# The softmaxed taps of a convolution built on every partition by VectorE instead of by a product, and two convolution steps of the second block placed ahead of the first gated product

## The reference, cut to what matters

```python
w = softmax(weight, axis=-1)               # weight: 8 heads x 7 taps, 1e-9 added to the sum
x = einsum('hk,bskhg->bshg', w, windows)   # out[s] = sum_k w[head, k] * x_pad[s + k]
h = sigmoid(x @ w_gate) * (x @ w_val)      # 192 -> 1536
x = h @ w_out                              # 1536 -> 192
r = maximum(x @ w_in2, 0)                  # 192 -> 2048
out = (r * r) @ w_out2                     # 2048 -> 192
```

## Time and profile before

| | |
|---|---|
| median of 3 runs | 2343.72 us (2342.58 to 2344.52) |
| the profiled execution, its own time | 2343.65 us |
| its span in the trace | 2341.9 us |
| TensorE (PE) busy | 2335.8 us, 100% of the span |
| VectorE (DVE) busy | 1884.9 us, 80% |
| ScalarE (ACT) busy | 1277.3 us, 55% |
| GpSimd (POOL) busy | 156.6 us, 7% |

### The profile page before, as it was taken

One profiled execution on the slowest core, in us unless ns is written; L12 is line 12 of the kernel. 1 busy time (PEld: TensorE's weight loads), 2 busy tenths in 40 slices (PEclk: granted clock), 3 DMA queues, 4 the chain that ended last, 5 costly groups with the idle time before them and its releaser, 6 DMA issues.

```text
span 2341.9 us, 54356 instructions
## 1 busy us (share of the span) xinstructions
PE 2335.8 (100%) x20539; PEld 1929.7 (82%) x20539; DVE 1884.9 (80%) x3968; ACT 1277.3 (55%) x2350; POOL 156.6 (7%) x125
## 2 busy tenths in 40 slices
PE   9999999999999999999999999999999999999999
PEld 7888888888888888888888888888888888888887
DVE  7778878788788787887878878788788787887856
ACT  5645555545554555544555545555555554455556
POOL 3100000000000000000000000000000000000000
PEclk9999999999999999999999999999999999999999
DMA  6111111011110111101111111111111111111101
GB/s 171 44 26 47 29 47 49 25 47 29 49 47 25 47 29 49 47 25 47 39 39 47 35 39 40 36 47 43 31 47 29 47 47 27 47 29 49 41 19 37
DMA packets 93343, 99.28 MB, mean 42 GB/s; under 512 B 8256, under 2 KB 77376, under 8 KB 93312
## 3 DMA queue, kind: packets, MB, share of 16 engines
q1 hardware_dynamic: 92240, 97.81, 16.7%
q10 hardware_dynamic: 1072, 1.05, 0.2%
HBM read 19.27 MB, written 12.58 MB: 14 GB/s over the span
## 4 chain that ended last, share of the span: by engine, by line
PE 99%; DVE 0%; issue 0%; ACT 0%; DVEq 0%; ACTq 0%
PE hp L506 55%; PE acc L571 25%; PE acc L579 17%; PE hp L507 1%; PE acc L572 0%; PE acc L580 0%; PE hp L681 0%; DVE y L1051 0%; PE hp L655 0%; DVE lo L1011 0%; DVE hid_t L997 0%; PE hp L516 0%; PE hp L628 0%; PE acc L671 0%; PE acc L506 0%
## 5 line engine op out<-in xcount | busy, mean ns | idle before, releaser
L506 PE MATMUL hp<-xs,w 64*128 64x512 f32 x5745 | 1394.5, 386 | 0.7 <-DVE hid_t L997 0.5
L507 PE MATMUL hp<-xs,w 64*128 64x512 f32 x5745 | 1394.5, 386 | 0.0
L506 PEld LDWEIGHTS hp<-xs,w 64*128 64x128 f32 x5745 | 1056.8, 184 | 227.3 <-DVE hid_t L997 1.8
L507 PEld LDWEIGHTS hp<-xs,w 64*128 64x128 f32 x5745 | 1056.8, 184 | 0.0
L1011 DVE TENSOR_TENSOR lo<-hid_t,hi 128x512 fp32r<-128x512 f32 x896 | 613.4, 688 | 63.9 <-ACT hi L777 59.8
L807 ACT ACTIVATE act_t<-hp 128x512 f32<-128x512 f32 x383 | 229.5, 599 | 690.4 <-PE hp L506 690.3
L572 PE MATMUL acc<-hi,wo 64*128 64x512 f32 x1788 | 547.7, 386 | 0.0
L571 PE MATMUL acc<-hi,wo 64*128 64x512 f32 x1788 | 547.7, 386 | 0.0
L810 ACT ACTIVATE act_t<-hp 128x512 f32<-128x512 f32 x512 | 302.8, 598 | 186.9 <-PE hp L507 186.8
L997 DVE TENSOR_TENSOR hid_t<-hp,act_t 128x512 f32<-128x512 f32 x383 | 264.4, 690 | 154.9 <-ACT act_t L807 146.6
L571 PEld LDWEIGHTS acc<-hi,wo 64*128 64x128 f32 x1788 | 329.0, 184 | 70.2
(11 more groups left out here) (116 smaller groups left out, 2175.4 us busy)
## 6 DMA issues: line engine op xcount, KB each, us to landing
xs<-xs SPq DMA_DIRECT2D x158, 256.0 KB, 3.8
xs<-y_rest SPq DMA_DIRECT2D x126, 128.0 KB, 3.4
out_dram<-stage SPq DMA_DIRECT2D x31, 384.0 KB, 2.6
xin<-in_x_dram SPq DMA_DIRECT2D x30, 384.0 KB, 3.3
moved<-y_parts SPq DMA_DIRECT2D x32, 128.0 KB, 2.2
moved<-z_parts SPq DMA_DIRECT2D x31, 128.0 KB, 2.2
stage<-in_moe_w_out_dram SPq DMA_DIRECT2D x7, 384.0 KB, 4.7
stage<-in_moe_w_in_dram SPq DMA_DIRECT2D x12, 128.0 KB, 2.8
```

The costliest lines, as they stand in the source:

```text
L506: low = pe.matmul(banks[:, 0, :], w[lower, wk, c], xs[lower, xk, :], start=s, stop=e)
L507: up = pe.matmul(banks[:, 1, :], w[upper, wk, c], xs[upper, xk, :], start=s, stop=e)
```

## The change

The raw `weight` goes to every partition by one transfer (56 numbers each, `heads_w`). `head_of` becomes a matrix of 128 partitions x 3 x 8 which holds a one where the partition's channel belongs to the head. VectorE multiplies the two (128 x 168), sums over the heads in two reductions, which leaves each channel's own raw taps on its partition, and works out the softmax there for both groups of channels at once (128 x 14). The product on TensorE, its wait and the copy out of PSUM are gone. `IDLE` goes from (5, 1, 1) to (5, 2, 1). ScalarE runs a sigmoid on one column ahead of the taps' one, and asks for its three weight pieces behind the arrival of `weight`. The steps of block 1's convolution stand ahead of `hidden` of tiles 0, 0, 2, 3, 6, 7, 8 (`TAPS_AHEAD`).

```diff
-    IDLE = (5, 1, 1)
+    IDLE = (5, 2, 1)
...
-        soft_w = sb("soft_w", [H, K])
-        exp_w = sb("exp_w", [H, K])
-        stat = sb("stat", [H, 4])
-        head_of = act_t[0:H, 0, 0:2 * P].rearrange("h (a c) -> h a c", a=2)
+        first_act = act_t[:].rearrange("p n c -> p (n c)")
+        heads_w = first_act[:, 0:H * K]
+        head_of = first_act[:, P:P + 3 * H].rearrange("p (a h) -> p a h", a=3)
+        picked = first_act[:, 2 * P:2 * P + 3 * H * K].rearrange("p (a h k) -> p a h k", a=3, h=H)
+        own_w, exp_w, rest_w = (act_t[:, 1, 2 * n * K:2 * (n + 1) * K].rearrange("p (t k) -> p t k", t=2) for n in range(3))
+        stat = act_t[:, 1, 6 * K:6 * K + 8].rearrange("p (n t) -> p n t", t=2)
...
-        TAPS_BEHIND = (5, 6)
+        TAPS_AHEAD = (0, 0, 2, 3, 6, 7, 8)
...
             idle(IDLE[0])
-            pe.wait_ge(heads, 8)
+            pe.wait_ge(heads, 7)
             turn_rest(0)
             idle(IDLE[1])
-            pe.wait_ge(soft, 8)
-            for tile in range(2):
-                pe.matmul(hp[:, tile, 0:K], head_of[:, tile, :], soft_w[:], start=True, stop=True) \
-                  .then_inc(taps_ready, 1)
             turn_main(0)
             idle(IDLE[2])
             first_taps()
...
-            act.dma_start(soft_w[:], weight).then_inc(w_conv_loaded, 16)
-            act.wait_ge(soft, 1)
-            act.activation(exp_w[:], soft_w[:], ACT.Sigmoid, bias=stat[:, 0:1]).then_inc(sig_w_done, 1)
+            act.dma_start(heads_w, weight.rearrange("(o h) k -> o (h k)", o=1).broadcast_to([P, H * K])) \
+               .then_inc(w_conv_loaded, 16)
+
+            act.wait_ge(zeroed, 1)
+            act.activation(first_act[:, N - 1:N], zeros[:, 0:1].bitcast(F32), ACT.Sigmoid)
+            act.wait_ge(w_conv_loaded, 16)
             for n in range(3):
+                if n == 2:
+                    act.wait_ge(soft, 5)
+                    act.activation(exp_w, rest_w, ACT.Sigmoid).then_inc(sig_w_done, 1)
                 src, p0, p1 = pieces[n][0][1]
                 act.dma_start(stage_of(n, p0, p1), src).then_inc(stage_loaded[n % STAGES], 16)
             xT_copy(0, 0)
...
                     if prev is None:
-                        if 2 <= t < K + 2 and t not in TAPS_BEHIND:
-                            conv_tap(j + 1, t - 2)
+                        for k, ahead in enumerate(TAPS_AHEAD):
+                            if t == ahead:
+                                conv_tap(j + 1, k)
...
-                    if prev is None and t in TAPS_BEHIND:
-                        conv_tap(j + 1, t - 2)
...
+            dve.wait_ge(heads, 4)
             dve.wait_ge(w_conv_loaded, 16)
-            dve.tensor_reduce(stat[:, 0:1], soft_w[:], AX.X, ALU.max, negate=True).then_inc(soft, 1)
+            of_heads = heads_w.rearrange("p (h k) -> p h k", h=H)
+            dve.tensor_tensor(picked, of_heads.unsqueeze(1).broadcast_to([P, 3, H, K]),
+                              head_of.unsqueeze(3).broadcast_to([P, 3, H, K]), ALU.mult).then_inc(soft, 1)
+            dve.wait_ge(soft, 1)
+            dve.tensor_reduce(own_w[:, 0, :], picked[:, 2, :, :].rearrange("p h k -> p k h"), AX.X, ALU.add) \
+               .then_inc(soft, 1)
+            dve.tensor_reduce(own_w[:, 1, :], picked[:, 0:2, :, :].rearrange("p a h k -> p k (a h)"), AX.X, ALU.add) \
+               .then_inc(soft, 1)
+
+            dve.wait_ge(soft, 3)
+            dve.tensor_reduce(stat[:, 0, :], own_w, AX.X, ALU.max, negate=True).then_inc(soft, 1)
+            dve.wait_ge(soft, 4)
+            dve.tensor_tensor(rest_w, own_w, stat[:, 0, :].unsqueeze(2).broadcast_to([P, 2, K]), ALU.add).then_inc(soft, 1)
             dve.wait_ge(sig_w_done, 1)
```

More of the change, by code:

```diff
@@ L160, in conv_gated_squared_mlp @@
         turn_begun = sem("turn_begun")
-        taps_ready = sem("taps_ready")
         conv_part = sem("conv_part")
@@ L437, in _ @@
             nc.gpsimd.memset(head_of, 1.0).then_inc(heads, 1)
[L438 to L450, removed]
+            pool.wait_ge(heads, 1)
+            nc.gpsimd.affine_select(out=head_of, in_=head_of, compare_op=ALU.is_ge, fill=0.0, base=P,
+                                    pattern=[[-R, 3], [-GROUP, H]], channel_multiplier=1).then_inc(heads, 1)
+            pool.wait_ge(heads, 2)
+            nc.gpsimd.affine_select(out=head_of, in_=head_of, compare_op=ALU.is_ge, fill=0.0, base=GROUP - 1 - P,
+                                    pattern=[[R, 3], [GROUP, H]], channel_multiplier=-1).then_inc(heads, 1)
+            pool.wait_ge(heads, 3)
+            nc.gpsimd.affine_select(out=head_of[:, 1, :], in_=head_of[:, 1, :], compare_op=ALU.is_ge, fill=0.0, base=-R,
+                                    pattern=[[0, H]], channel_multiplier=1).then_inc(heads, 1)
             nc.gpsimd.memset(ident[:], 1.0).then_inc(heads, 1)
-            pool.wait_ge(heads, 6)
+            pool.wait_ge(heads, 5)
             nc.gpsimd.affine_select(out=ident[:], in_=ident[:], compare_op=ALU.is_ge, fill=0.0, base=0,
                                     pattern=[[1, P]], channel_multiplier=-1).then_inc(heads, 1)
-            pool.wait_ge(heads, 7)
+            pool.wait_ge(heads, 6)
             nc.gpsimd.affine_select(out=ident[:], in_=ident[:], compare_op=ALU.is_ge, fill=0.0, base=0,
@@ L939, in _ @@
             xT_copy(0, 0)
-            act.wait_ge(heads, 8)
-            act.wait_ge(soft, 9)
+            act.wait_ge(heads, 7)
+            act.wait_ge(soft, 12)
             diagonal(0)
@@ L1211, in _ @@
             dve.memset(xT[:, :, 0:HALO], 0.0).then_inc(halo_ready, 1)
+            dve.wait_ge(heads, 4)
             dve.wait_ge(w_conv_loaded, 16)
-            dve.tensor_reduce(stat[:, 0:1], soft_w[:], AX.X, ALU.max, negate=True).then_inc(soft, 1)
-            dve.wait_ge(sig_w_done, 1)
[L1217 to L1225, removed]
+            of_heads = heads_w.rearrange("p (h k) -> p h k", h=H)
+            dve.tensor_tensor(picked, of_heads.unsqueeze(1).broadcast_to([P, 3, H, K]),
+                              head_of.unsqueeze(3).broadcast_to([P, 3, H, K]), ALU.mult).then_inc(soft, 1)
@@ L1226, in _ @@
+            dve.tensor_tensor(rest_w, own_w, stat[:, 0, :].unsqueeze(2).broadcast_to([P, 2, K]), ALU.add).then_inc(soft, 1)
+            dve.wait_ge(sig_w_done, 1)
+            dve.tensor_scalar(rest_w, exp_w, -1.0, 1.0, ALU.mult, ALU.add).then_inc(soft, 1)
             dve.wait_ge(soft, 6)
-            dve.reciprocal(stat[:, 3:4], stat[:, 2:3]).then_inc(soft, 1)
+            dve.reciprocal(rest_w, rest_w).then_inc(soft, 1)
             dve.wait_ge(soft, 7)
-            dve.tensor_scalar(soft_w[:], exp_w[:], stat[:, 3:4], None, ALU.mult).then_inc(soft, 1)
@@ L1230, in _ @@
-            dve.wait_ge(taps_ready, 2)
-            dve.tensor_copy(taps[:], hp[:, 0:2, 0:K]).then_inc(soft, 1)
+            dve.tensor_tensor(exp_w, exp_w, rest_w, ALU.mult).then_inc(soft, 1)
+            dve.wait_ge(soft, 8)
+            dve.tensor_reduce(stat[:, 1, :], exp_w, AX.X, ALU.add).then_inc(soft, 1)
             dve.wait_ge(soft, 9)
+            dve.tensor_scalar(stat[:, 2, :], stat[:, 1, :], 1e-9, None, ALU.add).then_inc(soft, 1)
+            dve.wait_ge(soft, 10)
+            dve.reciprocal(stat[:, 3, :], stat[:, 2, :]).then_inc(soft, 1)
@@ L1233, in _ @@
+            dve.wait_ge(soft, 11)
+            dve.tensor_tensor(taps[:], exp_w, stat[:, 3, :].unsqueeze(2).broadcast_to([P, 2, K]), ALU.mult) \
+               .then_inc(soft, 1)
+            dve.wait_ge(soft, 12)
             first_conv()
```

## The result

The changed kernel takes **2348.09 us** (median of 17 runs, 2346.49 to 2350.82) against 2343.64 (17 runs, 2342.00 to 2345.10) for the kernel before, a ratio of 1.0022 with an interval of 1.0015 to 1.0028. It is 4.45 us slower where 1.7 less was forecast, and it lies above the whole range (2340.3 to 2344.2). The profiled execution took 2349.78 with a span of 2348.0, against a span of 2341.9 before.

The account below looks back on a forecast made before the run. TensorE, busy 100% of the span, was taken as the bound. An earlier start (0.8) and fewer later stops (0.85) made 1.65 us off the profiled 2343.65, so 2342.0, range 2340.3 to 2344.2.

Parts of the forecast that it names:

- The transfer: At the start, `weight` to every partition: 1.8 us from issue, there at 2.6 (2.2 to 4.1).
- The sign that I had given myself: At the start: the prediction is wrong if the new transfer takes over 2.7 us.
- The slower rival: At the start: transfer lands behind x, at 5.0, tap products at 8.8; 0.6 us slower, 2344.3; chance 0.1.
- the 0.01 for more than 0.2% slower: Whole kernel: chance 0.01 of being slower by more than 0.2%, which is 4.7 us.
- VectorE's 3.0 from landing to taps: At the start: VectorE's taps ready 3.0 us after the transfer's landing.
- Moved steps: Block 1's convolution steps at new tiles: TensorE's later stops shrink, 0.85 us gained (bounds -0.35 to 1.3).
- the fourth tile's stop: TensorE's stop at the fourth tile grows by 0.35 us, the price of the new step order.
- the tenth's: TensorE's stop at the tenth tile, 0.76 us with refill, goes, with 0.9 to spare.
- meetings with GpSimd: VectorE and GpSimd shutting each other out: up to 1.2 us each; two more ahead of `hidden(7)` restore the 0.76 stop.
- The start's 0.8: At the start: TensorE's gated products begin 0.8 us earlier, the middle of 0.4, 0.8 and 1.6.
- the clock's step ahead of the tap products: At the start: fast clock comes before the tap products; 2.5 us off in all, 2341.2; chance 0.2.

Follow-up runs that it names:

- e5: Kernel before plus an unused transfer of 128 different 224-byte rows of x, first on ScalarE's queue: 2344.39 us against 2343.59.
- e11: The change, with each partition's 56 numbers read from 128 different rows of x instead of `weight`: 2341.74 us against 2343.62 for the kernel before.
- e1: The change with block 1's convolution steps back at their old tiles: 2348.55 us against 2343.70 for the kernel before.
- e3: The change with ScalarE asking for its three weight pieces at once, without waiting for `weight`: 2344.69 us against 2343.70 for the kernel before.
- e4: Kernel before plus an unused transfer of `weight`'s 224 bytes to 128 partitions, first on ScalarE's queue: 2348.70 us against 2343.59.
- e7: Kernel before plus an unused transfer of one 224-byte row of x, read 128 times: 2348.52 us against 2343.75.
- e9: Kernel before with ScalarE's three weight pieces asked for only after VectorE's softmax, no added transfer: 2346.12 us against 2343.75.
- e8: Kernel before plus an unused transfer of `weight`'s 224 bytes to 64 partitions: 2346.03 us against 2343.75.
- e2: Kernel before with only the new order of block 1's convolution steps: 2342.60 us against 2343.70.
- e10: Kernel before with only the new order of block 1's convolution steps, measured a second time: 2342.61 us against 2343.75.
- e12: The change with 128 different rows of x in place of `weight` and the weight pieces asked for at once: 2342.82 us against 2343.62 before.

## Why the prediction was wrong, point by point

**The transfer, the term that failed.** "It moves 28 KB and is nearer to the small one: I take 1.8, so it is there at 2.6 (2.2 to 4.1)." Measured: 4.3 us, VectorE starts at 5.22. Even the upper bound was too low. I bounded it by bytes, with the 256 KB of x as the far end, and the property that decides was in neither row: all 128 reads go to one place. With 128 different rows it takes 2.0 (e5, e11), with one row repeated 3.5 to 4.4 (e1, e3, e4, e7, the change). The sign that I had given myself, over 2.7 us for the transfer, was the right one. No row of the profile before had such a transfer, and that should have opened the range upwards, not closed it at the largest transfer in sight.

**It was priced alone.** The slower rival had it landing at 5.0, almost exactly what came, and worked out 2344.3, against 2348.09. It moved only the chain behind the landing (L681 to 8.8; it was 9.46), and left x where it was. The two parts of x came at 0.89 + 5.3 = 6.2 and 1.39 + 6.3 = 7.7, in place of 3.3 and 4.7, and TensorE stood 2.20 us for it. The window of 2 to 4 us shows it: 101 GB/s in place of 247 for everybody. A chance of 0.1 for that rival was too little, with "no row shows 128 such rows" beside it. So was the 0.01 for more than 0.2% slower, since no case had the parts together; the ratio is 1.0022.

**ScalarE's wait was not priced at all.** "nor do the two DMA issues ahead of it" looked at whether the requests delay the sigmoid, not at whether the wait delays the requests. Behind the added wait stood three transfers. They went out from 5.14 on instead of 2.42, behind block 1's x (3.81 and 4.44) and w_out (4.99) of the other queue, which before had all been issued after them, and landed 10.8 us later. ScalarE then waited 4.89 for the first, with `y_rest` and `xs` behind it. e9 gives 2.4 us for late requests alone, e3 gets 3.4 back. In the change this part comes only with the slow transfer: in e11 the same wait lets the requests go at 2.82 and costs nothing.

**The clock was priced for 20 products, not for the stream.** That TensorE's idle time could bring it down again was not among the cases. After 4.38 us of idle time it went at 1.2 GHz until 23.9, 2.1 us more by the twelfth pair. In e1 the same happened after 2.58 us. In e4, after 1.99, the first pairs went fast and those from 18.8 to 21.3 every 0.43 us (granted clock 0.53 from 18 to 20). In e7, with 1.78, the pairs still went every 0.23 us, and in e3, with 0.34, too. The times of the single executions go with the clock: in e1 the eight with a mean granted clock of 0.999 took 2348.4 to 2350.0 and the three at 1.000 2346.3 to 2347.1, and in e4 it is 2348.7 to 2350.1 and 2347.2 to 2348.1. In e8 the two groups don't part in this way. Of the change, 16 of 17 executions have 0.999, and of e3 none. So part of the 3.4 that e3 gets back is this clock.

**The rest of the steps held.** VectorE's 3.0 from landing to taps: 3.03. L728 is out. Moved steps, 0.85 forecast: 1.1 by the medians of e2 and e10, 1.2 by the traces of e10 and e11 from the first gated product to block 1, the fourth tile's stop 0.26 longer and the tenth's gone. As for meetings with GpSimd, the longest in the change, a step's two instructions in 2.66 us at 39.31 where they take 1.14 elsewhere, didn't bring back a stop at the tenth tile either; the kernel before had one as long, from 32.48 on. The start's 0.8: e11 less e10, both against their before, gives 1.88 - 1.14 = 0.7; by the one trace of e11 it is 1.23, with the clock's step ahead of the tap products. The size of this term held, and the reason that I gave for it didn't show.

**The best version of the same computation** among these is the step order alone (e2, e10), 2342.6: 1.1 us below before and 5.5 below the change.

**What stays open.** Why 64 copies take nearly as long as 128 while holding others back less. Why the weight pieces of the change needed 10.8 us where those of e9, late as well, needed 8.2: the window from 8 to 10 us has 126 GB/s in the change, and 136 to 155 in e1, e4 and e7, with the DMA engines fully busy, against 254 in e3, where the requests are early, and 240 in e9, where no row is repeated. Why the clock fell in one of these starts and not in another. And e12 against e11. A small copy of `weight` to 32 partitions, spread from there, was not tried, nor was reading it behind x.

## What to carry to other kernels

Before costing a broadcast from DRAM by its bytes, ask how many of its reads go to the same place: here with 32 it landed as soon as 128 different rows did, with 64 or more it was 1.3 to 2.4 us above, and with 128 it slowed the transfers of the other queue. When a change adds a wait to an engine, list the requests that stand behind that wait in its queue, and then what in the same engine's program stands behind their arrival. And measure a new transfer by itself in the old kernel first: e4, a few lines, would have shown a loss of this size before any of the rest was written.

## What the hardware showed that I had not expected

- One row of 224 bytes, read 128 times, landed after 3.5 to 4.4 us; 128 different rows of the same size after 2.0. Meanwhile, from 2 to 4 us, the core's DMA moved 99 to 113 GB/s (e7, the change, e4, e1) and 90 in e3, against 247, with its engines busy for only 0.40 to 0.49 of the time. With 64 copies it was 216 at 0.88.
- Transfers that were asked for 2.1 us later landed 4.7 us later (e9, by the medians of the three: 4.50 + 8.2 against 2.42 + 5.6). Block 1's x, asked for at 3.82 and 4.45, was ahead of them then; that this is what held them was not tried apart.
- The granted clock reads 1.00 from 2 to 4 us, where products of 512 columns go every 0.43 us, and 0.50 from 20 to 22, at the same pace. At the start of this kernel the starts of the products tell the pace, and the column doesn't.
